# Gated delta attention on one core: query grams and state sums in all four corners of the array, one piece per chunk

## What is computed

```
def _attn_ref(q, k, v, beta):
    k_n = k / (np.linalg.norm(k, axis=-1, keepdims=True) + 1e-06)
    for t in range(S):
        y[:, :, t] = np.einsum('bhd,bhde->bhe', q[:, :, t], state)
        v_old = np.einsum('bhde,bhd->bhe', state, kt)
        state = state + bt[:, :, :, None] * np.einsum('bhd,bhe->bhde', kt, vt - v_old)

def _moe_ref(x, w_in, w_out):
    h = x @ w_in
    return np.maximum(0.01 * h, h) @ w_out

def _moe2_ref(x, modality_id, w_gate, modality_bias, w1, w2):
    logits = x @ w_gate + modality_bias[modality_id]
    e_idx = np.argmax(logits, axis=1)
    ... for each expert e: out[mask] = gate_w[mask, None] * (np.maximum(x[mask] @ w1[e], 0.0) @ w2[e])
```

## Time and profile before

| | us |
|---|---|
| median of 3 runs | 978.0 |
| lowest, highest | 977.09, 982.07 |
| profiled execution, whole | 978.93 |
| its span, first to last instruction | 977.2 |
| TensorE matmuls busy in the span | 870.9 (89%) |
| VectorE busy | 553.5 (57%) |
| ScalarE busy | 350.6 (36%) |
| chain that ended last: TensorE | 67% |
| chain that ended last: VectorE | 15% |

### The profile page before, as it was taken

How to read it: one execution, slowest core, us unless ns; L and a number is a source line. 1 busy time by engine, 2 the same in 40 slices (tenths; PEclk the granted TensorE clock), 3 DMA queues, 4 the chain that set the end, 5 groups by cost and what they waited for, 6 DMA issues and landing times.

```text
span 977.2 us, 26906 instructions
## 1 busy us (share of the span) xinstructions
PE 870.9 (89%) x10528; PEld 766.0 (78%) x10529; DVE 553.5 (57%) x1578; ACT 350.6 (36%) x609; POOL 87.6 (9%) x100
## 2 busy tenths in 40 slices
PE   3775889989999998999989999999969999999962
PEld 3664678878888887888878888888759898889862
DVE  4974994588638862798359842344642333333350
ACT  3364335542545253444444342323411212121230
POOL 1000000000020002000100001010121212121210
PEclk9965899999999999999999999999999999999996
DMA  9904272345143533344153313255051111111122
GB/s 127 337 4 75 62 150 68 68 107 101 34 92 74 104 62 52 99 86 81 41 102 84 74 28 84 58 94 175 32 171 33 48 32 48 32 48 32 40 74 73
DMA packets 148308, 77.92 MB, mean 80 GB/s; under 512 B 112496, under 2 KB 144240, under 8 KB 147824
## 3 DMA queue, kind: packets, MB, share of 16 engines
q1 hardware_dynamic: 143264, 66.59, 30.4%
q0 software_dynamic: 4096, 9.48, 3.2%
q10 hardware_dynamic: 848, 0.39, 0.2%
HBM read 59.30 MB, written 13.21 MB: 74 GB/s over the span
## 4 chain that ended last, share of the span: by engine, by line
PE 67%; DVE 15%; ACT 7%; DMA 4%; issue 3%; SPq 1%; ACTq 1%; DVEq 0%; POOL 0%; POOLq 0%
PE bank L518 17%; PE bank L503 14%; PE bank L605 11%; PE bank L580 10%; DVE inv_t L1299 2%; DVE inv_tmp L1293 2%; PE bank L590 2%; PE bank L381 2%; PE bank L410 2%; ACT diag L987 2%; DVE g_raw L1368 1%; PE bank L484 1%; DVE tr L1305 1%; PE bank L471 1%; DVE inv_a L1255 1%
## 5 line engine op out<-in xcount | busy, mean ns | idle before, releaser
L518 PE MATMUL bank<-wo_hi,g_hi 128*128 128x392 f32 x384 | 139.1, 362 | 7.3 <-DVE g_lo L1373 4.0
L518 PE MATMUL bank<-wo_hi,g_lo 128*128 128x392 f32 x384 | 132.2, 344 | 0.0
L518 PE MATMUL bank<-wo_lo,g_hi 128*128 128x392 f32 x384 | 132.1, 344 | 0.0
L1368 DVE SCALAR_TENSOR_TENSOR g_raw<-g_raw 128x512 f32<-128x512 f32 x96 | 66.3, 691 | 105.0 <-ACT g_raw L1043 105.0
L503 PE MATMUL bank<-x_hi,wi_hi 128*128 128x512 f32 x288 | 118.3, 411 | 6.2 <-ACT g_raw L1043 3.4
L1043 ACT ACTIVATE g_raw<-bank 128x512 f32<-128x512 f32 x96 | 57.3, 597 | 170.5 <-PE bank L503 170.1
L503 PE MATMUL bank<-x_hi,wi_lo 128*128 128x512 f32 x288 | 114.0, 396 | 0.0
L503 PE MATMUL bank<-x_lo,wi_hi 128*128 128x512 f32 x288 | 113.9, 395 | 0.0
L1050 ACT ACTIVATE g_hi<-g_raw 128x512 fp32r<-128x512 f32 x96 | 60.7, 632 | 116.9 <-DVE g_raw L1368 116.9
L1373 DVE TENSOR_TENSOR g_lo<-g_raw,g_hi 128x512 fp32r<-128x512 f32 x96 | 66.3, 691 | 41.9 <-ACT g_hi L1050 41.7
L518 PEld LDWEIGHTS bank<-wo_hi,g_hi 128*128 128x128 f32 x384 | 72.7, 189 | 13.8 <-issue 6.0
(11 more groups left out here) (215 smaller groups left out, 1493.3 us busy)
## 6 DMA issues: line engine op xcount, KB each, us to landing
wo_lo<-wo_lo_d SPq DMA_DIRECT2D x80, 196.0 KB, 2.4
w_raw<-in_moe_w SPq DMA_DIRECT2D x6, 1536.0 KB, 8.4
x_rows<-stage SPq DMA_DIRECT2D x6, 770.0 KB, 6.2
kq_in_rows<-in_k SPq DMA_DIRECT2D x6, 768.0 KB, 7.0
k_raw<-in_k SPq DMA_DIRECT2D x24, 192.0 KB, 4.0
vals<-in_v SPq DMA_DIRECT2D x48, 96.0 KB, 2.9
kq_in_rows<-in_q SPq DMA_DIRECT2D x6, 768.0 KB, 8.8
x_raw<-y_t SPq DMA_DIRECT2D x33, 96.0 KB, 2.4
```

The source lines that it names most:

```text
L518: mm = pe.matmul(acc[i][:, 0:DX], g[f % 2][:, P * i:P * i + P], w, start=(f == 0 and k == 0), stop=(f == FT - 1 and k == 2))
L1368: dve.scalar_tensor_tensor(out=g_raw[f % 2][:], in0=g_raw[f % 2][:], scalar=0.01, in1=g_raw[f % 2][:], op0=ALU.mult, op1=ALU.max).then_inc ...
```

## The change

`gram_q` and `state_sum` take the form of `gram_k`: one call per chunk, pairs of odd number crosswise in a bank of their own. `gram_q(t, 0)` stays in f=15 and `gram_q(t, 1)` goes to f=0; nothing of it is left in f=1 and 2. `state_sum(t, 0)` stays in f=7, `state_sum(t, 1)` stands in f=12 wholly ahead of `down`. The even bank is evicted by one instruction over 128 partitions; the odd one by two over 64 partitions each, which bring the halves back to their own partitions (`halves`). `add_s` of chunk 1 moves ahead of `norm`, and in slot (-1, 12) also ahead of `split_x(0)`. `gram_q` now waits for all four pieces of the queries; before it waited for the two of its half. Matmuls stay as many, PSUM evictions of these two steps go from 8 to 12 per set.

```diff
-            def gram_q(t, m):
-                for i in range(2):
-                    pe.wait_ge(*is_drained(("QT", t, m % 2 * 2 + i)))
-                b, done = fill(("QK", t, m))
+            def gram_q(t, c):
+                for m in range(4):
+                    pe.wait_ge(*is_drained(("QT", t, m)))
+                to = [fill(("QK", t, c, odd)) for odd in range(2)]
                 for j in range(8):
...
+                    for odd in range(2):
+                        for hh in range(2):
+                            mm = pe.matmul(to[odd][0][half_p(hh ^ odd), CH * j:CH * j + CH], k_t[head_p(hh), 2 * j + odd, chunk(c)],
+                                           q_t[head_p(hh), 2 * j + odd, chunk(c)], start=True, stop=True)
...
-                    if f < 3:
-                        gram_q(n + 1, f + 1)
+                    if f == 0:
+                        gram_q(n + 1, 1)
...
-                        state_sum(n + 1, 1, 0)
+                        state_sum(n + 1, 1)
...
-                        state_sum(n + 1, 0, 0)
-                        state_sum(n + 1, 0, 1)
-                    if f == 12:
-                        state_sum(n + 1, 1, 1)
+                        state_sum(n + 1, 0)
...
+            def halves(odd):
+                return [(half_p(hh), half_p(1 - hh)) for hh in range(2)] if odd else [(slice(0, P), slice(0, P))]
+
+            def mask_q(t, c, odd):
+                dve.wait_ge(*is_filled(("QK", t, c, odd)))
+                for to, at in halves(odd):
+                    mm = dve.tensor_tensor(qk_t[to, every_other(c, odd), :], by_8(att_bank(("QK", t, c, odd))[at, :]),
+                                           mask[at, :].unsqueeze(1).broadcast_to([to.stop - to.start, 8, CH]), ALU.mult)
+                mm.then_inc(drain(("QK", t, c, odd)), 1)
...
+                for to, at in halves(odd):
+                    mm = dve.tensor_tensor(new[to, odd::2, :], old[to, odd::2, :], by_48(att_bank(("S", t, c, odd))[at, :]), ALU.add)
+                mm.then_inc(drain(("S", t, c, odd)), 1)
```

More of the change, by code:

```diff
@@ L401, in betas @@
                 mm.then_inc(s.beta_tp, 1)
-            def gram_q(t, m):
-                for i in range(2):
-                    pe.wait_ge(*is_drained(("QT", t, m % 2 * 2 + i)))
-                b, done = fill(("QK", t, m))
+            def gram_q(t, c):
+                for m in range(4):
+                    pe.wait_ge(*is_drained(("QT", t, m)))
+                to = [fill(("QK", t, c, odd)) for odd in range(2)]
                 for j in range(8):
-                    pair = m % 2 * 8 + j
-                    for hh in range(2):
-                        mm = pe.matmul(b[half_p(hh), CH * j:CH * j + CH], k_t[head_p(hh), pair, chunk(m // 2)],
-                                       q_t[head_p(hh), pair, chunk(m // 2)], start=True, stop=True)
-                mm.then_inc(done, 1)
+                    for odd in range(2):
+                        for hh in range(2):
+                            mm = pe.matmul(to[odd][0][half_p(hh ^ odd), CH * j:CH * j + CH], k_t[head_p(hh), 2 * j + odd, chunk(c)],
+                                           q_t[head_p(hh), 2 * j + odd, chunk(c)], start=True, stop=True)
+                        if j == 7:
+                            mm.then_inc(to[odd][1], 1)
             def merge_x(t, m):
@@ L460, in updates, with state_sum @@
                             mm.then_inc(to[odd][1], 1)
-            def state_sum(t, c, m):
-                if c == 0 and m == 0:
+            def state_sum(t, c):
+                if c == 0:
                     pe.wait_ge(s.k_in, 64 * t + 64)
@@ L466, in state_sum @@
                     pe.wait_ge(*is_drained(("U", t, c, odd)))
[L467 removed]
+                to = [fill(("S", t, c, odd)) for odd in range(2)]
                 for j in range(8):
[L469 to L473 removed]
+                    for odd in range(2):
+                        g = PAIRS * c + 2 * j + odd
+                        for hh in range(2):
+                            mm = pe.matmul(to[odd][0][head_p(hh ^ odd), HD * j:HD * j + HD], k_raw[half_p(hh), g, :], u_sb[half_p(hh), g, :],
+                                           start=True, stop=True)
+                        if j == 7:
+                            mm.then_inc(to[odd][1], 1)
             def outputs(t, c):
                 for m in range(2):
[L477 removed]
+                    pe.wait_ge(*is_drained(("QK", t, c, m)))
                     pe.wait_ge(*is_drained(("U", t, c, m)))
@@ L1334, in sub_w, with add_s @@
                 dve.tensor_tensor(x, x, by_48(att_bank(("W", t, c, odd))), ALU.subtract).then_inc(drain(("W", t, c, odd)), 1)
-            def add_s(t, c, m):
-                dve.wait_ge(*is_filled(("S", t, c, m)))
-                old, new = (state[i][:, eight(m), :].rearrange("p a b -> p (a b)") for i in (c, 1 - c))
-                dve.tensor_tensor(new, old, att_bank(("S", t, c, m))[:, 0:8 * HD], ALU.add).then_inc(drain(("S", t, c, m)), 1)
+            def add_s(t, c, odd):
+                dve.wait_ge(*is_filled(("S", t, c, odd)))
+                old, new = state[c], state[1 - c]
+                for to, at in halves(odd):
+                    mm = dve.tensor_tensor(new[to, odd::2, :], old[to, odd::2, :], by_48(att_bank(("S", t, c, odd))[at, :]), ALU.add)
+                mm.then_inc(drain(("S", t, c, odd)), 1)
             def split_wi(p):
@@ L1573, in slot @@
                         sub_w(n + 1, 1, 1)
+                if cur and f == 12:
+                    add_s(n + 1, 1, 0)
+                    add_s(n + 1, 1, 1)
                 if nxt:
@@ L1582, in slot @@
                         norm(n + 2)
-                if cur and f == 12:
-                    add_s(n + 1, 1, 0)
-                    add_s(n + 1, 1, 1)
                 for i in inv[len(inv) // 2:]:
```

19 lines of the change are left out of this document (5 added, 14 removed).

## The result

The changed kernel takes 985.27 us (median of 8 runs, 983.72 to 986.96), the kernel before 977.08 in the same series. The ratio is 1.0076, 95% interval 1.0054 to 1.0097: slower by 0.8%. Its profiled execution has a span of 983.4 us, 6.2 more than before.

What follows compares the result with a forecast made beforehand. TensorE sets the pace in slots 5 to 12, VectorE ends with it in 12 to 5. Head +3.9, f=7 -2.5, end -0.8, sets 2 to 5 0, clock +5.25: +5.9 on 978.93, 984.8; by the median 984, range 973 to 990.

Steps and rivals of the forecast that it cites:

- Pieces on TensorE: Query grams and state sums: a whole chunk in four corners costs what half did; grams save 2.4 us per set.
- Price of a moved half: VectorE's evictions over 64 partitions that move data cost a full one, about 0.69 us for masks, 0.55 for additions.
- the part of the gain that rested on half the price: Rival, chance 0.13: 64-partition evictions cost half, VectorE 1.7 us faster in slots 12 to 5, time 971.
- the dearer eviction: Rival, chance 0.11: moved halves cost more; a third more adds 1.1 us in each of six sets, 990; double, 1004.
- The new wait: `gram_q` in f=15, sets 2 to 5: TensorE idles 3.2 us for the fourth query piece, ending 1.9 us later.
- What is given back: Slots 1 to 5: VectorE's 2.0 us of waits for ScalarE's copies go, so `tr` moves by 0 (+-0.5) per set.
- Sets 0 and 1: VectorE is full there: two masks cost 1.2 us per set, slot (-1, 12) adds 1.5; +3.9 together.
- The clock: Granted clock falls behind three or four of the four new waits, 1.5 us each, about +5 us.
- f=7 and the end: Shorter state sums save 0.5 us in f=7 of five tiles, -2.5, and 0.8 in f=12 of the last set.
- The rule on copies as the bound: Rival from the skill: PSUM evictions on VectorE become the bound, the 3.3 us savings go too, time 987.

Runs made afterwards that it cites:

- one eviction: Changed kernel with odd banks emptied by one instruction over 128 partitions, halves left wrong; ratio to the kernel before 1.0494, unreadable since the third layer runs more blocks.
- the runs of the two parts alone: Kernel before with only the state sums in four corners, ratio 0.9997, and kernel before with only the grams in four corners, ratio 1.0060.
- mixed kernel: Changed kernel with the old form in all of set 0 and set 1's chunk 0 gram, and gram of chunk 0 behind `down` of f=15; ratio to before 0.9968.
- state sums alone: Kernel before with only the state sums in four corners and additions ahead of the norm, grams and masks as before; ratio 0.9997.
- evictions alone: Kernel before with every second piece of query grams and state sums evicted by two in-place instructions over 64 partitions; ratio 1.0074.
- the wait alone: Kernel before with only the query grams made to wait for all four pieces of the queries; ratio 1.0090.
- the head as before: Changed kernel with the old form up to the first gram of set 1, gram of chunk 0 still ahead of `down`; ratio to the kernel before 1.0052.
- the copies first: Changed kernel with ScalarE copying query pieces three and four in f=14 ahead of `round_g` and `split_x`; ratio to the kernel before 1.0023.
- the first four kernels: Kernel before with the longer wait only (1.0090), state sums only (0.9997) or grams only (1.0060) in four corners; changed kernel with query copies earlier (1.0023).

## Why the prediction was right

The time came out as forecast, 985.3 against 984.0, slower as forecast, and by the mechanism named: a new wait for the fourth piece of the queries, with the clock behind it, and evictions that cost their full price in the head. Some of the terms were off and made up for one another, so that the closeness of the number, 1.3 us, is in part luck: the head, the wait in set 2 and f=7, whose gain didn't come, went against the forecast, and the end, where 3 us came back in place of 1.3, and set 4 made up for them.

- **Pieces on TensorE.** Right. The sum of `L410` and the state sum is 30.2 us of matmul time, against 50.4 before, and L410 x64 takes 1.16 at the upper clock.
- **Price of a moved half.** Right: 689 and 553 ns, the nearest rows' price. So neither the part of the gain that rested on half the price nor the dearer eviction came about. Their number is another matter: for sets 2 to 5 the sum had 0 up to `tr`, with as many masks as before on that stretch, but the one eviction shows that without the moved halves these four sets would be some 5 us shorter. So evictions have a price there too, which stands against what TensorE saves. Set 3, without a fall of the clock in any of four traces, takes 101.7 and 102.4 us in the kernel before and 102.4 both times in the changed one.
- **The new wait.** Right for sets 3 to 5: 3.00, 3.00 and 2.98 us, where 3.2 was forecast, and the `down` of f=14 waits for VectorE as forecast, 1.0. Mis-sized for set 2: 5.87. There ScalarE's `x_hi` waits for the load of x, and the copies stand behind it on ScalarE. The step on the new wait was read in tile 1 (set 3) and carried over to sets 2 to 5, though the trace of the kernel before already has the late load. ScalarE's timeline, first before, then after:

```profile
209.88 1.49 ACT L1039 ACTIVATE x_hi<-x_raw 128x1536 fp32r<-128x1536 f32 x1 [2.10 <-DMA x_raw<-y_t]
...
216.58 1.48 ACT L1039 ACTIVATE x_hi<-x_raw 128x1536 fp32r<-128x1536 f32 x1 [2.23 <-DMA x_raw<-y_t]
217.97 1.06 ACT L978 ACTIVATE q_t<-bank 128x512 f32<-128x512 f32 x2
```

  That load holds up ScalarE in set 2 only among sets 2 to 5. With the longer idle the clock was at its lower level for 6.8 us, and set 2 lost 3.8 in the first pair of traces and 1.0 in the second, where about 0.8 stood in the sum (5.25 for the clock and -2.0 for f=7, over four sets).
- **What is given back.** It held: VectorE's waits for g_raw in the stretch of the earlier trace rows (331 to 354 us in the changed kernel) are down to 0.4 us in two places, from 2.0 in four, and set 3, with a wait of 3.00 and no fall of the clock, is 0.7 us longer in the first pair of traces and as long in the second. One effect wasn't foreseen: a shorter state sum makes the wait longer, as the runs of the two parts alone show (1.7 against 3.0 us).
- **Sets 0 and 1.** Forecast +3.9, measured +4.8 and +4.9, and +4.7 between the means of all traces. Two waits weren't foreseen: the gram of chunk 1 in slot (0, 0) waits 4.07 us for the masks of chunk 0; and `up` of the first slot waits 3.62 for x_lo. The first costs nothing that can be seen: the mixed kernel has it too, 4.32 us, and its merge of set 1 is where that of the kernel before is.

```profile
99.61 0.77 PE L506 MATMUL bank<-x_hi,wi_hi 128*128 128x512 f32 x1 [3.62 <-DVE x_lo L1372]
...
115.70 1.56 PE L410 MATMUL bank<-q_t,k_t 48*64 48x64 f32 x48 [4.07 <-DVE qk_t L1315]
```

- **The clock.** Three or four falls at 1.5 us were forecast; three came, one of them twice as long. In set 4 the kernel before had a stall of 2.49 with a fall of its own, so that the difference there is -1.1. In the second trace of the kernel before, neither that stall nor the fall is there: it was chance, which the forecast took as it stood. The forecast also added its falls to a trace that had two of its own in these sets and took none of them off.
- **f=7 and the end.** Forecast -2.5 and -0.8; the state sums alone give 0.9997, so nothing of the -2.5 shows. The new waits for g_lo aren't in f=7 itself: in the changed kernel sets 3 to 5 have them in slot 14 (1.0) and slot 1 (0.3), so I read it as time that TensorE gains in f=7 and waits away in slot 14, which no run tests by itself. Behind the last merge about 3 us came back instead of 1.3, and that repeats: the stretch took 422.0 and 422.3 us in two traces of the kernel before, 419.2 and 419.3 in two of the changed one. Why it is more than forecast is open.
- **The rule on copies as the bound.** The Trainium skill, TensorEngine Tiling (Array Packing), section PSUM Bottleneck, says that packing leaves the emptying of PSUM as it was. The traces agree for the head (evictions alone, +3.9 us up to the merge of set 1) and, against what I wrote, in part beside the network (one eviction, 6.7 us less over sets 2 to 5). For f=7 the ratio of 0.9997 fits the rule but doesn't show it. By it alone I had 987; the measured 985.3 lies between that and the forecast.

**What stays open:** why evictions alone cost 0.7% and the wait alone 0.9%, when the two together, with shorter matmuls, cost 0.8%. The parts may overlap, since a wait for the copies gives VectorE time to catch up, but no run shows that, and the stalls without a shown cause and the falls of the clock behind them are as large as what would have to be told apart.

## What to carry to other kernels

Packing matmuls into four corners brings their time down to little over half (the two steps from 50.4 to 30.2 us) and adds evictions, and it joins two steps into one, which must then wait for the inputs of both: ask which copy is last for the joined step, and what stands ahead of it in its engine's queue. Take the form only in stages in which the evicting engine has time, and don't read that from its busy share (VectorE is busy 71% of the time between the merges of sets 1 and 5, and the evictions still cost time there), and put a step with a late input behind independent matmuls of the same slot. Where two engines end together, the order of small steps on the second is worth as much as the matmuls saved on the first.

## What the hardware showed

- A fall of the granted clock isn't fixed by the idle time ahead of it. Waits of 2.98 to 3.04 us at the same place of the program, with the same work around them, had a fall with them in sets 4 and 5 of all four traces that have them (the changed kernel twice, the one eviction, the head as before), and in set 3 only in the last of the four. With the copies first, waits of 2.02 and 2.03 us had one behind them in all of sets 3 to 5.
- An instruction of VectorE that reads one half of the partitions and writes the other costs what one in place costs: 689 ns moved, 684 ns in place for 64x512 (evictions alone, L1314).
- TensorE idles without a shown cause up to 3.26 us, mostly in the outputs of a set or in the key gram beside them, with another length in each trace. On the chip of the first four kernels all four traces have such stalls, of about 0.4 us or more, in the outputs of each of sets 2 to 5, two to four to a set. Such a stall and the 3.3 us at half the clock behind it are some 5 us, as much as most of the effects studied here.
